# Attention rows scaled before they are turned, with the inverse row sums spread across partitions by two DMA steps

## The chip, the cores and the metric

One core of one Trainium2 chip runs the whole program. The metric is device time in microseconds. The engines are named as in the profile: PE (TensorE, with PEld for its weight loads), DVE (VectorE), ACT (ScalarE), POOL (GpSimd), SP (SyncE, which here only issues DMAs and waits).

## The reference, cut to what matters

Three blocks run one after the other: windowed attention (2 batches, 8 heads, 768 tokens, head dimension 64), a token-mixing and channel MLP, and a gated MLP with a spatial product. The change touches only the end of the attention block and the hand-over to the second block.

```
scores = scale * q @ k^T + bias          # -1e9 outside the window of 96 and the 8 global keys
a = exp(scores - max(scores))
a = a / (sum(a) + 1e-9)
x = (a @ v) as [batch, token, head*dim]
u = x + ((x^T @ U) @ V)^T                # then ch = relu(u @ w_ch1) @ w_ch2; u + ch; the third block
```

## The kernel before

The attention is cut into 24 **quads**: quad g is query tile t = g // 2 (128 queries) with four heads (g % 2 picks which). A tile sees its own block of 128 keys and the block before it (with the global keys copied into it); the first tile of each batch (quads 0, 1, 12, 13) sees one block only. The heads of a quad are held as two pairs m = 0, 1, and within a pair e = 0, 1.

The order is written out by hand: each engine runs a loop over steps s = -2 to 23 (DVE to 24), and in step s handles several quads at different depth.

- PE, step s: `turn(s)` transposes the probabilities of quad s, `turn_o(s-1)` transposes the head outputs of quad s-1, `turn_x(s-2)` transposes the scaled rows of quad s-2 back, `scores(s+2)` makes the scores of quad s+2, then in single steps `gather_z` (s = 13), `fold_z` (14) or a `mix` (15, 17, 19, 21), and `weigh(s)` multiplies with v into `o_bank`.
- DVE, step s: `take_oT(s-1)` copies `o_bank` (dims on partitions, queries along the row) to SBUF, `take_probT(s)` copies half of the turned probabilities, `take_x(s-1)` multiplies the once-turned output in `aux` (queries on partitions) by the inverse sums into `x_all`, `invert(s)` makes the reciprocal of the four sums per query, `score_bias(s+2)` adds the bias and takes the row minimum.
- ACT, step s: `take_probT(s)` (the other half), `add_eps(s+1)` adds 1e-9 to the sums, `take_xT(s-2)` copies the twice-turned output from `aux` into `uT` (dims on partitions), `exps(s+2)` makes the exponentials and their row sums.
- POOL splits the q and k of later quads into high and low parts (`split_qk`) and copies the global keys and values.
- SP loads: `load_qk(t)` issues two DMAs of 256 KB for one tile, `load_v(t)` one. All of them are issued as soon as their buffer is free. After the attention loop it goes on to `load_stage(n)` for the weights from n = 2 on.

So the sums of a query lie on the query's partition, and the output of `weigh` has the dims on partitions; that is why before, the output is turned, scaled and turned again. `x_all` (queries on partitions) is needed for `gather_z`, `uT` (dims on partitions) for all that follows. After step 23 PE runs `hidden(0)`, the first product of the second block; from there to the end 402 us of the span follow.

Of the kernel before, what the change touches and what calls it, by code (L numbers as in the profile page):

```python
# [13 lines left out]
P = 128  # L14
# [11 lines left out]
def build(nc, qk, qT, kT, v, cfg, U, V, w_ch, w_in, w_spT, b_sp, w_out, x_dram, out):  # L26
    B, DM, S = qT.shape
    D = 64
# [22 lines left out]
    with ExitStack() as ctx:  # L51
# [95 lines left out]
        for name, shape, dtype in (("cfg_i", [P, 4], I32), ("cfg_f", [P, 4], F32), ("row_min", [P, 8], F32),  # L147
                                   ("row_sum", [P, 16], F32), ("row_one", [P, 16], F32), ("row_inv", [P, 8], F32),
# [14 lines left out]
        oT = [at(f"oT{r}", [P, 2, P], F32, SLOT * 11 + 2048 + 1024 * r) for r in range(2)]  # L163
# [18 lines left out]
        def sem(name):  # L182
# [15 lines left out]
        sum_eps, inv_ok = sem("sum_eps"), sem("inv_ok")  # L198
        probT_d, probT_a, pv_done, x_half = sem("probT_d"), sem("probT_a"), sem("pv_done"), sem("x_half")
        oT_sb, o_ps = sem("oT_sb"), sem("o_ps")  # L200
        xT_ps, xT_sb, z_acc, z_round, z_split = [sem(n) for n in ("xT_ps", "xT_sb", "z_acc", "z_round", "z_split")]
# [19 lines left out]
            sem("wide_" + n) for n in ("turned", "probT", "out_ps", "o", "store", "back", "heads")]  # L221

# [18 lines left out]
        z_bank, fold_bank = (s_bank[0], aux), (s_bank[2], aux)  # L241

        def mix_bank(j):

            if j < FIRST:

                return s_bank[0]
            return o_bank if j >= 2 * KD and j % 2 else aux

        OT_AMID = (0, 1, 12)
# [112 lines left out]
        def _(sp):  # L365
# [44 lines left out]
            with sp.If(near):  # L410
# [9 lines left out]
                load_v(TILES - 1)  # L420
# [37 lines left out]
        def _(pool):  # L458
# [191 lines left out]
            with pool.If(near):  # L650
# [7 lines left out]
                for g in range(QUADS):  # L658
# [14 lines left out]
                    if g >= 17 and g % 2:  # L673
                        split_u((g - 17) // 2)
# [35 lines left out]
        def _(dve):  # L710
# [62 lines left out]
            def invert(g):  # L773
                sums = row_one[:, g % 4 * 4:g % 4 * 4 + 4]
                dve.wait_ge(sum_eps, g + 1)
                if g >= 2:
                    dve.wait_ge(x_half, g - 1)
                vec.reciprocal(row_inv[:, g % 2 * 4:g % 2 * 4 + 4], sums).then_inc(inv_ok, 1)

            def take_oT(g):  # L780
                dve.wait_ge(pv_done, g + 1)
                if g >= 2:
                    dve.wait_ge(o_ps, g - 1)
                vec.tensor_copy(oT[g % 2][:], o_bank[:, 0:2 * P].rearrange("p (c q) -> p c q", c=2)).then_inc(oT_sb, 1)

            def take_x(g):
                t, hq = divmod(g, 2)
                inv = row_inv[:, g % 2 * 4:g % 2 * 4 + 4]
                dve.wait_ge(inv_ok, g + 1)
                dve.wait_ge(o_ps, g + 1)  # L790
                if g:
                    dve.wait_ge(xT_ps, g)
                if t == XS:
                    dve.wait_ge(z_acc, 1)
                cols = slice(hq * 256, hq * 256 + 256)
                vec.tensor_tensor(x_all[:, t % XS, cols].rearrange("p (h d) -> p h d", d=D),
                                  aux[:, 0:256].rearrange("p (h d) -> p h d", d=D),
                                  inv.unsqueeze(2).to_broadcast([P, 4, D]), ALU.mult).then_inc(x_half, 1)
# [69 lines left out]
            with dve.If(near):  # L868
                for s in range(-2, QUADS + 1):
                    if s >= 1 and s - 1 not in OT_AMID:  # L870
                        take_oT(s - 1)
                    if 0 <= s < QUADS and s != 2:
                        take_probT(s)
                    if s >= 1:
                        take_x(s - 1)
                    if 0 <= s < QUADS:
                        invert(s)
                    if s in OT_AMID:
                        score_bias(s + 2, 0)
                        take_oT(s)  # L880
# [5 lines left out]
                    if s == 14:  # L886
                        split_z(0)
                    if s in (15, 17, 19):
                        sum_u((s - 15) // 2)
                    if s == 22:  # L890
                        sum_u(FIRST - 1)
            with dve.Else():
# [12 lines left out]
                dve.sem_inc(x_half, QUADS)  # L905
# [244 lines left out]
        def _(act):  # L1150
# [19 lines left out]
            def exps(g, half=None):  # L1170
                w = P * blocks(g // 2)
                if g >= 4:
                    act.wait_ge(x_half, g - 3)
# [9 lines left out]
            def add_eps(g):  # L1183
                q = g % 4 * 4
                act.wait_ge(expd, 2 * g + 2)
                sc.activation(row_one[:, q:q + 4], row_sum[:, q:q + 4], ACT.Copy, bias=1e-9).then_inc(sum_eps, 1)

# [7 lines left out]
            def take_xT(g, after=0):  # L1195

                t, hq = divmod(g, 2)
                act.wait_ge(xT_ps, g + 1)
                if after:
                    act.wait_ge(x_half, after)  # L1200
                sc.activation(uT[:, 2 * hq:2 * hq + 2, t * P:(t + 1) * P],
                              aux[:, 2 * P:4 * P].rearrange("p (k t) -> p k t", k=2), ACT.Copy).then_inc(xT_sb, 1)
# [54 lines left out]
            with act.If(near):  # L1257
                for s in range(-2, QUADS):
                    if s >= 3:
                        take_probT(s)  # L1260
                    if s == 13:
                        split_stage(0)
                        copy_z(0)
                    if 0 <= s + 1 < QUADS:
                        add_eps(s + 1)
                    if s == 14:
# [5 lines left out]
                    if s >= 2:  # L1272
# [704 lines left out]
```

## Time and profile before

| | |
|---|---|
| median of 3 runs | 494.83 us (494.77 to 494.99) |
| span of the profiled execution, first to last instruction | 493.2 us |
| PE busy | 489.0 us (99% of the span) |
| DVE, ACT, POOL busy | 310.2, 222.0, 250.2 us |
| granted TensorE clock | 1.000 over the span |

The span leaves out what lies before the first and after the last instruction; the profile gives no time of its own for that, and the median of the runs lies 1.6 us above the span. Busy shares are of the span. Steps of the attention are best read by the start of the same PE instruction in two neighbouring steps.

### The profile page before, as it was taken

To read this page: it belongs to the slowest core of one execution; us is meant where nothing else is said; L and a number is where in the kernel's file an instruction comes from. 1 tells how busy PE (TensorE), PEld (TensorE's weight loads), DVE (VectorE), ACT (ScalarE), POOL (GpSimd) and SP (SyncE) were. 2 spreads that over 40 slices of the span, in tenths; PEclk is the share of its full clock that TensorE was granted. 3 is DMA by queue.
4 is the path that set the end of the run, shared out by engine and by line. 5 is a ranking of instruction groups with operands and counts; after the bars stand their busy time and mean duration, and the time that the engine had idled before them with its cause. 6 is when DMAs were issued, how large, how long until landed. Compare 5 with 4: busy or idle time off the path is not lost.

```text
span 493.2 us, 7961 instructions
## 1 busy us (share of the span) xinstructions
PE 489.0 (99%) x2804; PEld 409.3 (83%) x2804; DVE 310.2 (63%) x727; ACT 222.0 (45%) x520; POOL 250.2 (51%) x221
## 2 busy tenths in 40 slices
PE   9999999999999999999999999999999999999997
PEld 8788677887888888888888888888888888998986
DVE  5888788421279456564655656557868888878600
ACT  7988889532234633242332322415433356333122
POOL 5997576443346666854566546232885201950000
PEclk9999999999999999999999999999999999999999
DMA  8734501132222322012222020220213000001022
GB/s 236 236 127 111 191 2 45 46 128 86 81 87 89 129 85 71 31 72 85 85 86 78 8 85 3 84 64 2 64 65 115 4 0 1 1 1 43 23 85 108
DMA packets 14697, 36.29 MB, mean 74 GB/s; under 512 B 2496, under 2 KB 2752, under 8 KB 14656
## 3 DMA queue, kind: packets, MB, share of 16 engines
q1 hardware_dynamic: 12640, 32.35, 19.8%
q10 hardware_dynamic: 2016, 3.41, 1.8%
q8 instruction: 24, 0.39, 0.3%
q14 instruction: 17, 0.14, 0.1%
HBM read 32.61 MB, written 3.15 MB: 72 GB/s over the span
## 4 chain that ended last, share of the span: by engine, by line
PE 82%; DVE 6%; POOL 4%; ACT 3%; issue 2%; DVEq 2%; DMA 1%; SPq 0%; ACTq 0%
PE bank L1792 15%; PE bank L1724 9%; PE bank L1644 9%; PE bank L1874 8%; PE bank L1821 8%; PE bank L1814 8%; PE bank L1513 7%; PE bank L1551 4%; PE bank L1569 4%; PE bank L1536 4%; PE bank L1503 1%; POOL sp_op L587 1%; PE bank L1583 1%; DVE newton L1020 1%; DVEq L1008 1%
## 5 line engine op out<-in xcount | busy, mean ns | idle before, releaser
L532 POOL TENSOR_TENSOR w_slot<-stage,w_slot 128x1024 fp32r<-128x1024 f32 x30 | 73.0, 2445 | 65.4 <-ACT w_slot L1249 65.4
L940 DVE TENSOR_TENSOR uT<-bank,uT 128x512 f32<-128x512 f32 x68 | 45.8, 689 | 25.2 <-PE bank L1821 23.2
L1179 ACT ACTIVATE prob<-prob,row_min 128x256 f32<-128x256 f32 (+1 forms) x96 | 45.9, 480 | 6.9 <-DVE row_min L756 6.8
L1792 PE MATMUL bank<-u_op,s_slot 128*128 128x512 f32 x192 | 47.6, 389 | 0.0
L1724 PE MATMUL bank<-hid,w_slot 128*128 128x512 f32 x192 | 46.9, 393 | 0.0
L1644 PE MATMUL bank<-u_split,w_slot 128*128 128x512 f32 x192 | 46.5, 391 | 0.0
L1814 PE MATMUL bank<-hid,w_slot 128*128 128x512 f32 x192 | 46.1, 389 | 0.0
L1821 PE MATMUL bank<-hid,w_slot 128*128 128x512 f32 x192 | 46.1, 389 | 0.0
L978 DVE TENSOR_TENSOR part<-part,bank 128x512 f32<-128x512 f32 x40 | 27.4, 686 | 26.9 <-PE bank L1792 26.5
L1724 PEld LDWEIGHTS bank<-hid,w_slot 128*128 128x128 f32 x192 | 35.7, 188 | 8.2 <-issue 0.9
L1814 PEld LDWEIGHTS bank<-hid,w_slot 128*128 128x128 f32 x192 | 36.0, 188 | 7.5
L1821 PEld LDWEIGHTS bank<-hid,w_slot 128*128 128x128 f32 x192 | 36.0, 188 | 7.5
L1792 PEld LDWEIGHTS bank<-u_op,s_slot 128*128 128x128 f32 x192 | 36.0, 188 | 7.5
L1644 PEld LDWEIGHTS bank<-u_split,w_slot 128*128 128x128 f32 x192 | 35.7, 188 | 7.5 <-issue 0.2
L1249 ACT ACTIVATE w_slot<-stage 128x1024 fp32r<-128x1024 f32 x32 | 33.3, 1052 | 12.7 <-DMA stage<-in_w_ch 12.7
L756 DVE CUSTOM_DVE_ANT_0 prob<-bank,bias 128x256 f32<-128x256 f32 (+1 forms) x96 | 32.9, 398 | 6.4 <-PE bank L1536 5.5
L1792 PE MATMUL bank<-u_op,w_slot 128*128 128x512 f32 x144 | 36.5, 389 | 0.0
L950 DVE SCALAR_TENSOR_TENSOR hid<-bank,hid 128x512 fp32r<-128x512 f32 x16 | 11.1, 691 | 39.2 <-ACT hid L1307 39.0
L579 POOL TENSOR_TENSOR s_slot<-s_raw,s_slot 128x1024 fp32r<-128x1024 f32 x8 | 19.2, 2402 | 32.5 <-ACT s_slot L1254 32.5
L1910 PE MATMUL bank<-in_slot,y_split 128*128 128x512 f32 x144 | 32.8, 389 | 0.0
L1513 PE MATMUL bank<-y_split,in_slot 128*128 128x512 f32 x144 | 32.8, 389 | 0.0
L1792 PEld LDWEIGHTS bank<-u_op,w_slot 128*128 128x128 f32 x144 | 27.0, 188 | 5.6
(152 smaller groups left out, 963.5 us busy)
## 6 DMA issues: line engine op xcount, KB each, us to landing
stage<-in_w_ch SPq DMA_DIRECT2D x32, 512.0 KB, 3.3
qk_raw<-in_qk SPq DMA_DIRECT2D x23, 256.0 KB, 4.7
v_all<-in_v SPq DMA_DIRECT2D x12, 256.0 KB, 5.2
out_dram<-o_stage ACTq DMA_DIRECT2D x11, 256.0 KB, 2.0
stage<-in_w_spT SPq DMA_DIRECT2D x6, 384.0 KB, 3.1
stage<-in_w_in SPq DMA_DIRECT2D x4, 512.0 KB, 4.2
stage<-in_w_out SPq DMA_DIRECT2D x2, 512.0 KB, 4.0
V_raw<-in_V SPq DMA_DIRECT2D x4, 96.0 KB, 4.6
```

The costliest lines, as they stand in the source:

```text
L532: nc.gpsimd.tensor_tensor(dst[:, LO, :], stage[n % 2][:, 0:w], dst[:, HI, :].bitcast(F32), ALU.subtract).then_inc(w_lo, 1)
L756: last = vec.tensor_tensor_reduce(prob[r][:, e, 0:w], s_bank[2 * (g % 2) + e][:, m * KC:m * KC + w], bias0[:, h, :] if w == P else bias[:, ...
L940: vec.tensor_tensor(y, y_bank(e)[:], y, ALU.add).then_inc(y_sum, 1)
L1179: last = sc.activation(prob[r][:, e, 0:w], prob[r][:, e, 0:w], ACT.Exp, bias=row_min[:, k:k + 1], scale=-1.0, accum_out=row_sum[:, q:q + 1])
L1249: sc.activation(dst[:, HI, :], stage[n % 2][:, 0:w], ACT.Copy).then_inc(w_hi, 1)
L1513: last = mm(out_ap, lhs(a), rhs(c), start=(n == 0), stop=(n == 3 * len(terms) - 1))
L1644: last = mm(h_bank[f % 2][:], w_slot[f][:, a, k * P:(k + 1) * P], u_split[:, m, k, :], start=(k == 0 and p == 0), stop=(k == KD - 1 and p ...
L1724: last = mm(c_bank[k][:], w_slot[f][:, a, 512 + k * P:512 + (k + 1) * P], hid[f % 2][:, m, :], start=(f == 0 and a == HI and m == HI), sto ...
L1792: last = mm(seven_bank[held][:], lhs, u_op[op][:, m, k, :], start=not more and k == 0 and p == 0, stop=k == 1 and p == 2, skip_group_check ...
L1814: mm(y_bank(e + k)[:], w[r][:, a, 512 + k * P:512 + (k + 1) * P], hid2[r][n][:, m, :], start=(a == HI and m == HI), stop=False, skip_group ...
L1821: last = mm(y_bank(e + k)[:], w[r][:, a, 512 + k * P:512 + (k + 1) * P], hid2[r][n][:, m, :], start=False, stop=(a == LO), skip_group_chec ...
L1874: last = mm(s_banks(q)[held][:, 0:HT], lhs, sp_op[j][:, m, SP_AT[op], :], start=not more and j == 0 and n == 0, stop=j == TC - 1 and n == ...
```

## The change

- `turn_o` and `take_oT` are gone. Quads write alternately into `o_bank` and `aux` (`x_bank(g)`). DVE's `scale_x(g)` multiplies that bank, dims on partitions, by a tile `inv_rows[g % 3]` that holds the inverse sums along the row, the same for all dims of a head, and writes `uT` directly. PE's `turn_x(g)` turns `uT` back into the same bank, and ACT's `take_x(g)` copies it into `x_all`.
- The inverse sums lie on partitions and have to come to lie along the row on all partitions. SP does that through a scratch tensor in device memory: `store_inverse(g)` writes the 128 x 4 values, one element at a time since the target is transposed ("k q -> q k"); `spread_inverse(g)` waits until that has landed and issues two DMAs, each of which reads 2 x 128 values once for each of 64 partitions.
- SP's loads are interleaved with these: in the order store, spread, then `load_qk(g/2 + 4)` after each even quad up to 14, `load_v` at quads 1, 3, and from 11 on, and the first two weight loads at quad 6.
- `add_eps` leaves ACT. DVE's `invert` adds the 1e-9 itself right ahead of the reciprocal, and runs one quad earlier, in step g-1.
- PE's `weigh(g)` now waits for `x_half` of quad g-2 (ACT's `take_x`) instead of `oT_sb` of quad g-1. `gather_z`, `fold_z` and three of the four `mix` sit one step later (14, 15, and 16, 18, 20, 20).

```diff
+            def store_inverse(g):
+                sp.wait_ge(inv_ok, g + 1)
+                sp.dma_start(inv_dram[g, :, :].rearrange("k q -> q k"), row_inv[:, g % 4 * 4:g % 4 * 4 + 4],
+                             allow_slow_non_contiguous=True).then_inc(inv_out[g % 2], 16)
+            def spread_inverse(g):
+                sp.wait_ge(inv_out[g % 2], 16 * (g // 2 + 1))
+                if g >= 3:
+                    sp.wait_ge(xT_sb, g - 2)
+                for e in range(2):
+                    rows = slice(e * D, (e + 1) * D)
+                    sp.dma_start(inv_rows[g % 3][rows, :, :],
+                                 inv_dram[g, 2 * e:2 * e + 2, :].partition_broadcast(D)
+                                 ).then_inc(inv_in[g % 3], 16)
...
-                for t in range(3, TILES):
-                    load_qk(t)
-                    load_v(t - 1)
-                    if t == 6:
+                load_qk(3)
+                load_v(2)
+                load_v(3)
+                for g in range(QUADS):
+                    if g == 11:
+                        load_v(NT)
+                    store_inverse(g)
+                    spread_inverse(g)
+                    if g % 2 == 0 and g // 2 + 4 < TILES:
+                        load_qk(g // 2 + 4)
+                    if g in (1, 3):
+                        load_v((g + 7) // 2)
+                    if g % 2 and g >= 11 and (g + 3) // 2 < TILES:
+                        load_v((g + 3) // 2)
+                    if g == 6:
                         load_stage(0)
                         load_stage(1)
...
             def invert(g):
+                dve.wait_ge(expd, 2 * g + 2)
+                vec.tensor_scalar(row_one[:, q], row_sum[:, q], 1e-9, None, ALU.add).then_inc(sum_eps, 1)
+                if g >= 4:
+                    dve.wait_ge(inv_out[g % 2], 16 * (g // 2 - 1))
                 dve.wait_ge(sum_eps, g + 1)
-                vec.reciprocal(row_inv[:, g % 2 * 4:g % 2 * 4 + 4], sums).then_inc(inv_ok, 1)
+                vec.reciprocal(row_inv[:, q].rearrange("p (e m) -> p m e", e=2),
+                               row_one[:, q].rearrange("p (m e) -> p m e", e=2)).then_inc(inv_ok, 1)
+            def scale_x(g):
+                dve.wait_ge(inv_in[g % 3], 32 * (g // 3 + 1))
                 dve.wait_ge(pv_done, g + 1)
+                vec.tensor_tensor(x_tile(g), x_bank(g)[:, 0:256].rearrange("p (c q) -> p c q", c=2),
+                                  inv_rows[g % 3][:], ALU.mult).then_inc(xT_sb, 1)
...
                 for s in range(-2, QUADS + 1):
-                    if s >= 1 and s - 1 not in OT_AMID:
-                        take_oT(s - 1)
                     if 0 <= s < QUADS and s != 2:
                         take_probT(s)
                     if s >= 1:
-                        take_x(s - 1)
-                    if 0 <= s < QUADS:
-                        invert(s)
+                        scale_x(s - 1)
+                    if 0 <= s + 1 < QUADS:
+                        invert(s + 1)
...
+            def take_x(g):
+                act.wait_ge(x_ps, g + 1)
+                sc.activation(x_all[:, t % XS, hq * 256:hq * 256 + 256], x_bank(g)[:, 0:256],
+                              ACT.Copy).then_inc(x_half, 1)
...
             def weigh(g):
-                if g:
-                    pe.wait_ge(oT_sb, g)
+                if g >= 2:
+                    pe.wait_ge(x_half, g - 1)
...
                     if s >= 0:
                         turn(s)
-                    if s >= 1:
-                        turn_o(s - 1)
                     if s >= 2:
-                        pe.wait_ge(x_half, s - 1)
                         turn_x(s - 2)
```

## Rows read from the trace of the kernel before

**Rows 1.** The page's busy times, then stretches: busy us per engine, granted clock, DMA.
```profile
PE 489.0 (99%) x2804; PEld 409.3 (83%) x2804; DVE 310.2 (63%) x727; ACT 222.0 (45%) x520; POOL 250.2 (51%) x221
...
17.00:45.00 28.00, 27.87 (x324) 23.26 (x326) 23.50 (x98) 24.50 (x96) 26.63 (x37) 1.00 0.38 122
57.00:92.00 35.00, 34.93 (x375) 27.51 (x373) 28.96 (x108) 30.44 (x105) 23.50 (x32) 1.00 0.13 47
```
**Rows 2.** Timeline of PE: start us, us, engine, line, operation.
```profile
36.43 0.44 PE L1583 MATMUL bank<-ident,oT 128*128 128x128 f32 x2
36.71 0.38 PE L1591 MATMUL bank<-ident,x_all 128*128 128x128 f32 x2
37.02 0.97 PE L1536 MATMUL bank<-qk_split 64*128 64x256 f32 x12
37.92 1.09 PE L1569 MATMUL bank<-probT,v_all 128*64 128x128 f32 x16
...
40.48 0.97 PE L1536 MATMUL bank<-qk_split 64*128 64x256 f32 x12
...
92.15 3.02 PE L1644 MATMUL bank<-u_split,w_slot 128*128 128x512 f32 x12
```
**Rows 3.** Timeline of DVE in the same step.
```profile
37.23 0.42 DVE L796 TENSOR_TENSOR x_all<-bank,row_inv 128x256 f32<-128x256 f32 x1 [0.25 <-PE bank L1591]
37.57 0.17 DVE L778 RECIPROCAL row_inv<-row_one 128x4 f32<-128x4 f32 x1
38.03 0.43 DVE L756 CUSTOM_DVE_ANT_0 prob<-bank,bias 128x256 f32<-128x256 f32 x1 [0.30 <-PE bank L1536]
```
**Rows 4.** Timeline of ACT, from this step into the next.
```profile
38.91 0.51 ACT L1179 ACTIVATE prob<-prob,row_min 128x256 f32<-128x256 f32 x1 [0.53 <-DVE row_min L756]
...
40.89 0.58 ACT L1193 ACTIVATE probT<-bank 128x512 f32<-128x512 f32 x1
41.37 0.19 ACT L1186 ACTIVATE row_one<-row_sum 128x4 f32<-128x4 f32 x1
41.46 0.36 ACT L1201 ACTIVATE uT<-bank 128x256 f32<-128x256 f32 x1
```
**Rows 5.** Timeline of ACT at the start.
```profile
9.77 0.18 ACT L1179 ACTIVATION_READ_ACCUMULATOR prob<-prob,row_min 128x1 f32 x1
```
**Rows 6.** DMA issues of the page: KB each, median us from issue to landing.
```profile
qk_raw<-in_qk ACTq DMA_DIRECT2D x1, 256.0 KB, 3.5
out_dram<-o_stage ACTq DMA_DIRECT2D x2, 128.0 KB, 1.7
U_sb<-in_U SPq DMA_DIRECT2D x1, 96.0 KB, 5.2
cfg_i<-in_cfg SPq DMA_DIRECT2D x1, 2.0 KB, 3.0
```
**Rows 7.** The tile v_all: all landings of its loads.
```profile
DMA to landing us min/median/max: 2.6/5.2/6.0
```
**Rows 8.** Timeline of SP: its own time to issue.
```profile
3.54 0.57 SPq L408 DMA_DIRECT2D U_sb<-in_U  x1
...
9.13 0.43 SPq L385 DMA_DIRECT2D v_all<-in_v  x1
...
43.02 0.33 SPq L385 DMA_DIRECT2D v_all<-in_v  x1
43.40 0.91 SPq L377 DMA_DIRECT2D qk_raw<-in_qk  x2
```
**Rows 9.** DMA packets in 7.00 to 8.25 us, then in 451.8 to 452.7 us.
```profile
DMA packets 950, 0.42 MB, mean 338 GB/s; under 512 B 791, under 2 KB 791, under 8 KB 950
...
DMA packets 144, 0.26 MB, mean 291 GB/s; under 512 B 16, under 2 KB 16, under 8 KB 144
```
**Rows 10.** DMA activity from 53.5 to 59.0 us, in 40 slices of 0.14 us, and its issues.
```profile
DMA  0400000289968555236897855678998997662221
...
qk_raw<-in_qk SPq DMA_DIRECT2D x2, 256.0 KB, 3.5
```

More of the change, by code:

```diff
@@ L161, in build @@
         z_part = at("z_part", [P, DM], F32, SLOT * 11)
-        oT = [at(f"oT{r}", [P, 2, P], F32, SLOT * 11 + 2048 + 1024 * r) for r in range(2)]
+        inv_rows = [at(f"inv_rows{r}", [P, 2, P], F32, SLOT * 11 + 2048 + 1024 * r) for r in range(3)]
         pos_w = SLOT * 11 + 2048
@@ L672, in _ @@
                         split_early(1, g // 22)
-                    if g >= 17 and g % 2:
-                        split_u((g - 17) // 2)
+                    for j in range(FIRST):
+                        if g == MIX_AT[j] + 2:
+                            split_u(j)
             with pool.Else():
@@ L885, in _ @@
                         score_bias(s + 2)
-                    if s == 14:
+                    if s == 15:
                         split_z(0)
[L888 to L891, printed above, removed]
+                    for j in range(FIRST):
+                        if s == MIX_AT[j]:
+                            sum_u(j)
             with dve.Else():
@@ L1193, in take_probT, with wide_take_xT @@
                 sc.activation(probT[(2 * g + 1) % 4][:, 0:w], pt_bank[1][:, 0:w], ACT.Copy).then_inc(probT_a, 1)
-            def take_xT(g, after=0):
+            def take_x(g):
                 t, hq = divmod(g, 2)
[L1198 to L1202, printed above, removed]
+                act.wait_ge(x_ps, g + 1)
+                if t == XS and hq == 0:
+                    act.wait_ge(z_acc, 1)
+                sc.activation(x_all[:, t % XS, hq * 256:hq * 256 + 256], x_bank(g)[:, 0:256],
+                              ACT.Copy).then_inc(x_half, 1)
+            def wide_take_xT(g):
+                act.wait_ge(w_xT_ps, g + 1)
+                sc.activation(x_tile(g), x_bank(g)[:, 0:256].rearrange("p (k t) -> p k t", k=2),
+                              ACT.Copy).then_inc(w_xT, 1)
             def copy_z(b):
@@ L1262, in _ @@
                         split_stage(0)
+                    if s == GATHER:
                         copy_z(0)
-                    if 0 <= s + 1 < QUADS:
-                        add_eps(s + 1)
-                    if s == 14:
+                    if s >= 2:
+                        take_x(s - 2)
+                    if s == GATHER + 1:
                         round_z(0)
@@ L1271, in _ @@
                         set_bias(6)
-                    if s >= 2:
-                        take_xT(s - 2, s)
                     if s == 1:
@@ L1282, in _ @@
                         split_stage(1)
-                    if s in (16, 18, 20, 22):
-                        round_u((s - 16) // 2)
+                    for j in range(FIRST):
+                        if s == MIX_AT[j] + 1:
+                            round_u(j)
             with act.Else():
@@ L1294, in _ @@
                 for g in range(2 * NT):
-                    take_xT(g)
+                    wide_take_xT(g)
                 copy_z(0)
@@ L1299, in _ @@
                     round_u(j)
-                for g in range(2 * NT, QUADS - 2):
-                    take_xT(g)
+                for g in range(2 * NT, QUADS):
+                    wide_take_xT(g)
+                act.wait_ge(w_xT, QUADS)
+                act.sem_inc(xT_sb, QUADS)
+                act.sem_inc(x_half, QUADS - 2)
             for f in range(FT):
@@ L1315, in _ @@
                 if f == 0:
-                    take_xT(QUADS - 2, QUADS)
+                    take_x(QUADS - 2)
                 if f == 1:
-                    take_xT(QUADS - 1)
+                    take_x(QUADS - 1)
                 if f == 4:
@@ L1697, in _ @@
                 for g in range(2 * NT):
[L1698 to L1700 removed]
+                    wide_turn_x(g)
                 pe.wait_ge(U_in, 16)
@@ L1711, in _ @@
                 pe.wait_ge(w_back, 16 * TILES)
-                for g in range(2 * NT, QUADS - 1):
-                    pe.wait_ge(xT_sb, g)
-                    turn_x(g)
+                for g in range(2 * NT, QUADS):
+                    wide_turn_x(g)
                 pe.sem_inc(scored, QUADS)
@@ L1717, in _ @@
                 hidden(0)
+                turn_x(QUADS - 2)
             def contract(f):
```

121 lines of the change are left out of this document (51 added, 70 removed).

## The prediction

> **What bounds the kernel now.** First the busy times: PE is busy 99% of the span at a granted clock of 1.00, in the attention too (27.87 of 28.00 us, 34.93 of 35.00) [rows 1]. So the end is set by how much PE has to do, and a saved PE instruction is worth its time as long as nothing else takes its place. Next the timelines of one step, to see how much room the others have. PE needs 40.48 - 37.02 = 3.46 us for a step of two blocks, without a gap: 0.28 `turn_o`, 0.31 `turn_x`, 0.90 `scores`, and 1.97 `weigh` and `turn` together [rows 2]. DVE idles 0.25 ahead of `take_x` and 0.30 ahead of `score_bias`, both for PE [rows 3]; ACT idles 0.53 for DVE's row minimum [rows 4]. Then SP, which has nearly nothing to do before: it issues loads in 0.33 to 0.46 us each and never waits for one to land [rows 8]. `hidden(0)` starts at 92.15 [rows 2]; everything from there on is the same work in both kernels, so the forecast is made on this start.
>
> **What the change takes off.** PE loses two transposes per quad: from the start of `turn_o` to that of `turn_x` 0.28 us [rows 2], times 24 = 6.7 us at most. DVE loses `take_oT` (a copy of 128x256 as large as the 0.42 multiply [rows 3], about 0.34 from start to start, since instructions overlap) and gets a 128x4 add, bounded by the reciprocal's 0.17 from above [rows 3] and nothing from below; I take 0.1. ACT loses 0.09 per quad (41.37 to 41.46) and has a copy of the same size instead of `take_xT` [rows 4]. The multiply now reads its second operand from a full tile rather than a broadcast; same size, same price. `gather_z`, `fold_z`, `mix` only move by a step.
>
> **What it puts on ACT and PE.** `weigh(s)` now waits for `take_x(s-2)`, which ACT runs behind `take_probT(s)`, behind `exps(s+1)`. In the rows, `scores` end and `weigh` starts at 37.92; the exponentials that hang on them start at 38.91, `take_probT` follows at 40.89, the copy would start where `add_eps` stands, at 41.37, and take 0.36 [rows 2, 4]. With 0.11 for a signal (37.92 to DVE's 38.03 [rows 2, 3]) that is 3.92 us after the scores. PE without `turn_o` would be at its next `weigh` after 3.46 - 0.28 = 3.18 us. PE thus waits, and the wait closes a loop over two steps: (3.92 + 3.18) / 2 = 3.55 us per step, against 3.46. So in a plain step of two blocks the 0.28 saved is spent on ACT's copy and 0.09 more; steps with a `gather_z`, `fold_z` or `mix` between scores and `weigh`, and those with one block, keep the saving. Some 14 steps at +0.09 and 10 at -0.28 give -1.5 us; `invert(0)` ahead of `score_bias(1)` makes DVE wait for `exps(0)`, which end at 9.95 [rows 5], about +1 at the start. Without the DMAs the change would be worth about -0.5 us, and -6 at best.
>
> **What it puts on SP.** This is where I expect the time to be decided. SP waits inside its own loop: issue the store, wait until it has landed, issue two reads, then the loads, then the next quad's store. Nothing of the next quad is issued before. One round is
>
> - the store, issue to landing. The nearest row is a 128 KB store, 1.7 us [rows 6]. A 256 KB store moves 144 packets, 0.26 MB, within 0.9 us [rows 9], so about 0.4 of the 1.7 is data and 1.3 is there at any size. This store has 512 elements of 4 bytes, each a write of its own. Nothing before writes so small. `U_sb` is the nearest: of its 128-byte pieces, 791 small packets passed in 1.25 us beside other loads [rows 9], 1.6 ns each, so 512 take 0.8: 2.1 us. Lower bound 1.6 (the elements nearly free). Upper bound from the same load: 768 pieces landed 5.2 us after issue [rows 6], so at most 6.8 ns each, 3.5 for 512: 4.8 us. I take 2.1, since the measured passage is the closer case.
> - a signal, 0.11, and two issues of 0.33 to 0.43 [rows 8], 0.76: together 3.0 us per round.
>
> PE's loop needs scale of quad g only two steps after its inverse, 6.9 us, and one trip is 2.1 + 0.1 + 0.4 + 2.6 (the fastest 256 KB load [rows 7], for a 64 KB read) = 5.2. The latency alone would be hidden, then. But SP's rounds also carry the loads, and these cost twice: their issue, and the queue. Small transfers wait behind large ones of the same queue: `U_sb`, 96 KB, issued at 3.54 behind 256 KB loads, moved only after 7 us and landed after 5.2, where 256 KB alone lands in 2.6 [rows 6, 7, 8, 9]. A load's first packets go about 0.9 after its issue (53.55 to about 54.4, slice 7 [rows 10]) and it is done moving at about 2.3, so a store issued right behind it, which could start 0.9 after its own issue, is held back by 2.3 - 0.43 - 0.9 = 0.95 us, likewise after a pair (issued in 0.91 [rows 8], done at 2.75). The landing of 3.5 in another place [rows 10] would make it 1.85. I take 0.95.
>
> - 22 rounds, quads 0 to 21 (the last that PE needs ahead of `hidden(0)`): 22 x 3.0 = 66
> - eight `load_qk` in them: 8 x (0.91 + 0.95) = 14.9
> - eight `load_v`: 8 x (0.43 + 0.95) = 11.0
> - two weight loads of 512 KB at quad 6: 1 MB at the 338 GB/s of [rows 9] = 3.1
> - the first store stands behind the loads of the start, the last of which was already out at 9.13 before and comes at about 9.6 now [rows 8], and lands with them at about 14.5 instead of 12.5: 2.0
>
> The sum is 97.0 us, 4.4 per quad against PE's 3.46: SP is the new bound, and PE, DVE and ACT wait for `inv_in`. The inverse of quad 0 is ready at 9.95 + 0.45 = 10.4. Then 10.4 + 97.0 = 107.4; the last reads land 2.2 later (second issue at 0.38, 2.6 to land, 0.76 counted): 109.6; `scale_x` 0.53, `turn_x` 0.31, `take_x` 0.47, `weigh` 1.1: 112.0. Before it was 92.15: +19.9 us. On the profiled execution 493.2 + 19.9 = 513.1 us of span; the runs lie 1.6 above it, so 514.7, and I say **515 us**.
>
> **A rule beside it.** The store's fixed part is 1.3 us by [rows 6, 9]. The Trainium skill, page "DMA: Bandwidth & Descriptors", section "Anatomy of one DMA — SWDGE (gpsimd) path", gives some 2.0 us fixed plus bytes over 436 GB/s for a DMA of that path, mostly the receipt of the write; by it the store is 2.0 whatever its pieces, and the sum would be 2 us shorter, 513. The same page, "Rules for kernel authors", says that a strided last dimension lowers to one descriptor per element and should be rearranged; it gives no price per element, and no row here shows such a store.
>
> **The rivals.**
> 1. *Full gain.* If the store takes the lower 1.6 us and small writes slip past the loads, a pair of rounds with a load is 2 x 2.5 + 0.9 = 5.9, under PE's 6.9, and SP is hidden. If ACT also gets `take_x` done in time, because DVE with 0.24 us less to do feeds it earlier, the 6.7 us less 1 at the start come out: 489 us. Against: `U_sb` did not slip past, and DVE's start hangs on `scores`, not on its own work (its 0.30 wait [rows 3]).
> 2. *SP hidden, ACT's copy in the loop.* As 1, but with the 3.55 us step: -0.5, 494.3 us; from 493 to 496 by how many steps keep their saving. For it: the rows of ACT; against: all that speaks for SP's rounds. SP decides from a mean round of 3.5 us on, which is a store of 1.3 us with all the loads' costs, or of 2.6 with none.
> 3. *Costly element writes.* With the store above 3.1 us the sum passes 536 us, and at the upper bound of 4.8 it is 22 x 2.7 = 59 more, 574.
>
> **How the numbers follow.** Forecast 0.54 (its own range 500 to 536: store 1.6 to 3.1 us, loads' queueing from half of what I count to all); costly writes 0.12; ACT's loop 0.15; full gain 0.19. A measurement can tell 0.2%, 1 us. Faster: full gain and about half of case 2, 0.26. Same: 0.07 of case 2. Slower 0.67. The range reaches down to most of the full gain and up to where costly writes begin: 490 to 536.
>
> **What would show it.** Right: SP's own row of waits names the store's landing, about 2 us each, 24 times, and DVE's waits name the spread for `scale_x`, in sum near 20 us; PE's step in 20 to 50 us is 4 to 5 us rather than 3.46, shortest in the late quads without loads; `hidden(0)` starts near 112. `store_inverse` lands in about 2.1 alone and 3 behind a load. The granted clock stays at 1.00; should it fall where PE now has gaps, the time is above mine. Wrong: step 3.2 and no wait for DMA (rival 1), or step 3.55 with PE waiting ahead of `weigh` for ACT's copy into `x_all` (rival 2). The weakest terms are the store's 0.8 us for 512 elements and the 0.95 us behind each load; each 0.1 us on a round is 2.2 us in the end.

## The result, and the profile after

The changed kernel takes 689.4 us (median of 4 runs, 687.5 to 694.0) against 494.8 us: slower by a factor of 1.394, 95% interval 1.390 to 1.399. The forecast was 515 us, range 490 to 536. The direction and the place were right, the size was not: +195 us instead of +20.

The page of the profile after; its line of busy times answers to that of [rows 1]:

```profile
span 692.2 us, 7862 instructions
...
PE 545.1 (79%) x2756; PEld 447.7 (65%) x2756; DVE 305.3 (44%) x727; ACT 219.4 (32%) x496; POOL 250.4 (36%) x221
...
PE 58%; DMA 33%; SPq 6%; ACT 1%; issue 1%; DVE 0%; DVEq 0%; ACTq 0%
DMA inv_scratch<-row_inv 32%; PE bank L1816 11%; PE bank L1541 9%; PE bank L1750 7%; PE bank L1898 6%; PE bank L1838 6%; PE bank L1845 6%; PE bank L1674 6%; PE bank L1934 5%; SPq L412 4%; DMA inv_rows<-inv_scratch 1%; SPq L389 1%; SPq L397 1%; PE bank L1531 1%; ACT prob L1204 1%
```

The last two lines are the chain that ended last, by engine and by line. A third of the span is now a DMA, and nearly all of it is one: the store of the inverse sums into the scratch (`inv_scratch<-row_inv`). The waits and the DMA issues say the same from the other end:

```profile
SPq L412 <- DMA inv_scratch<-row_inv: 217.5, 24, 11.1
...
DVE uT L827 <- DMA inv_rows<-inv_scratch: 215.4, 24, 11.7
...
inv_rows<-inv_scratch SPq DMA_DIRECT2D x48, 64.0 KB, 4.0
inv_scratch<-row_inv SPq DMA_DIRECT2D x24, 2.0 KB, 9.5
```

SP stands 24 times, 217.5 us in all, until a store has landed (L412 is `spread_inverse`; L402 is `store_inverse`, L389 and L397 the loads of q and k and of v), and DVE stands 215.4 us ahead of `scale_x` (L827) for the spread. The store takes 9.5 us from issue to landing. One round of SP, from its timeline:

```profile
43.12 1.09 SPq L412 DMA_DIRECT2D inv_rows<-inv_scratch  x2
44.25 1.06 SPq L389 DMA_DIRECT2D qk_raw<-in_qk  x2
45.35 0.43 SPq L402 DMA_DIRECT2D inv_scratch<-row_inv  x1
55.33 2.12 SPq L412 DMA_DIRECT2D inv_rows<-inv_scratch  x2
```

Store issued at 45.35, the spread of the same quad at 55.33: 10 us in which SP issues nothing else. For the next quad's inverse SP waits once in the whole kernel, 0.8 us, so its rounds run back to back. What the DMA engines do from 48 to 56 us, in 40 slices of 0.2 us:

```profile
DMA  9955210000000000000000000000900000000000
...
DMA packets 614, 0.17 MB, mean 21 GB/s; under 512 B 539, under 2 KB 539, under 8 KB 613
```

The small packets are through by 49.2 us. Then the engines report nothing (one slice of other traffic aside), and the landing comes at 55.3. So the packets themselves are cheap, as I had read from `U_sb`; six microseconds lie behind the last of them. That they are the completion of the writes is a reading: the trace shows only the silence and the landing.

`hidden(0)`, at 92.15 before [rows 2], and what follows it (PE's timeline):

```profile
278.98 4.99 PE L1674 MATMUL bank<-u_split,w_slot 128*128 128x512 f32 x12
283.81 0.38 PE L1610 MATMUL bank<-ident,uT 128*128 128x128 f32 x2
283.94 1.85 PE L1674 MATMUL bank<-u_split,w_slot 128*128 128x512 f32 x7
288.81 1.30 PE L1674 MATMUL bank<-u_split,w_slot 128*128 128x512 f32 x5 [3.02 <-issue]
294.80 0.66 PE L1610 MATMUL bank<-ident,uT 128*128 128x128 f32 x2 [4.69 <-DVE uT L827]
```

It starts 186.8 us later. Another 12.2 us are lost behind it (the spans differ by 199.0), all of them in these rows. The spreads of the last quads are still under way: PE waits 4.69 us for `scale_x`, and 3.02 us for something that the profile does not name. The other 4.5 us are products of the second block that run at a lower clock: the first twelve take 4.99 us instead of 3.02 [rows 2] (granted 0.57 from 278.90 to 284.00 us), the twelve from 295.11 take 5.42 (0.51 from 295.00 to 300.40). From 300.40 on the granted clock is 1.00. Over the attention:

```profile
12.00:290.00 278.00, 139.82 (x868) 105.16 (x868) 63.97 (x276) 69.19 (x239) 61.47 (x84) 0.59 0.22 41
```

The trace agrees in so far as this store of 2 KB takes 9.5 us where one of 128 KB took 1.7 [rows 6]; the size of the writes alone does not explain it, since the experiments below have the same 512 writes done in 2.9 us elsewhere.

### The profile page after: what moved, and what is told of

It is laid out like the page before. It is cut to its first block, busy times and chain, and to the rows that moved or that the text cites. A ratio compares the mean times of both kernels' runs of the same rounds, so it can differ in the third digit from the quotient of the medians.

```text
span 692.2 us, 7862 instructions
## 1 busy us (share of the span) xinstructions
PE 545.1 (79%) x2756; PEld 447.7 (65%) x2756; DVE 305.3 (44%) x727; ACT 219.4 (32%) x496; POOL 250.4 (36%) x221
## 4 chain that ended last, share of the span: by engine, by line
PE 58%; DMA 33%; SPq 6%; ACT 1%; issue 1%; DVE 0%; DVEq 0%; ACTq 0%
DMA inv_scratch<-row_inv 32%; PE bank L1816 11%; PE bank L1541 9%; PE bank L1750 7%; PE bank L1898 6%; PE bank L1838 6%; PE bank L1845 6%; PE bank L1674 6%; PE bank L1934 5%; SPq L412 4%; DMA inv_rows<-inv_scratch 1%; SPq L389 1%; SPq L397 1%; PE bank L1531 1%; ACT prob L1204 1%
## 5 line engine op out<-in xcount | busy, mean ns | idle before, releaser
L827 DVE TENSOR_TENSOR uT<-bank,inv_rows 128x256 f32<-128x256 f32 x24 | 10.2, 424 | 215.4 <-DMA inv_rows<-inv_scratch 215.4
L1610 PE MATMUL bank<-ident,uT 128*128 128x128 f32 x48 | 16.2, 440 | 94.3 <-DVE uT L827 94.3
L1610 PEld LDWEIGHTS bank<-ident,uT 128*128 128x128 f32 x48 | 6.9, 201 | 102.5 <-DVE uT L827 97.2
L1599 PE MATMUL bank<-probT,v_all 128*64 128x128 f32 x352 | 42.0, 411 | 38.2 <-ACT x_all L1221 27.7
L1599 PEld LDWEIGHTS bank<-probT,v_all 128*64 128x64 f32 x352 | 33.2, 214 | 46.8 <-issue 32.5
L1674 PE MATMUL bank<-u_split,w_slot 128*128 128x512 f32 x192 | 48.6, 403 | 3.0 <-issue 3.0
L1750 PE MATMUL bank<-hid,w_slot 128*128 128x512 f32 x192 | 49.4, 408 | 0.0
L542 POOL CAST qk_split<-qk_split 128x128 fp32r<-128x128 f32 x16 | 4.6, 290 | 122.6 <-PE bank L1566 122.6
L1838 PE MATMUL bank<-hid,w_slot 128*128 128x512 f32 x192 | 46.1, 389 | 0.0
L1845 PE MATMUL bank<-hid,w_slot 128*128 128x512 f32 x192 | 46.1, 389 | 0.0
L1674 PEld LDWEIGHTS bank<-u_split,w_slot 128*128 128x128 f32 x192 | 37.3, 197 | 11.4 <-issue 3.6
L1566 PE MATMUL bank<-qk_split 64*128 64x256 f32 (+1 forms) x288 | 36.2, 412 | 7.8 <-DVE uT L840 6.0
L1566 PEld LDWEIGHTS bank<-qk_split 64*128 64x128 f32 x288 | 30.1, 299 | 15.1 <-issue 12.5
```

The costliest lines, as they stand in the source:

```text
L1566: last = mm(s_bank[2 * (g % 2) + e][:, m * KC:m * KC + w], qk_split[rows, a, c, Q, own], qk_split[rows, k, c, K, keys], start=(p == 0), st ...
L1599: last = mm(x_bank(g)[e * D:(e + 1) * D, m * P:(m + 1) * P], v_all[:, i - n + 1 + j, h * D:(h + 1) * D], probT[(2 * g + m) % 4][:, (e * n ...
L1674: last = mm(h_bank[f % 2][:], w_slot[f][:, a, k * P:(k + 1) * P], u_split[:, m, k, :], start=(k == 0 and p == 0), stop=(k == KD - 1 and p ...
L1750: last = mm(c_bank[k][:], w_slot[f][:, a, 512 + k * P:512 + (k + 1) * P], hid[f % 2][:, m, :], start=(f == 0 and a == HI and m == HI), sto ...
L1838: mm(y_bank(e + k)[:], w[r][:, a, 512 + k * P:512 + (k + 1) * P], hid2[r][n][:, m, :], start=(a == HI and m == HI), stop=False, skip_group ...
L1845: last = mm(y_bank(e + k)[:], w[r][:, a, 512 + k * P:512 + (k + 1) * P], hid2[r][n][:, m, :], start=False, stop=(a == LO), skip_group_chec ...
```

## The experiments

### Is it the number of writes, their size, or their place?

**e1_runs16.** The scratch is written in runs of 16 bytes:

```diff
-  inv_dram[g, :, :].rearrange("k q -> q k")
+  inv_dram[g, :, :].rearrange("k q -> (k q)").rearrange("(q k) -> q k", k=4)
```

> The store writes the same 2 KB of a quad as 128 runs of 16 bytes instead of 512 single elements (the scratch then holds them in another order, so the scaling is by misplaced values); all waits and all other transfers are as in the changed kernel. Theory: the landing of the store (9.5 us median in the changed kernel, while its packets move in about 1.2 us) is made of its many small writes, each completed after the other, about (9.5 - 1.3) / 512 = 16 ns each. Then 128 writes land in about 1.3 + 2.0 = 3.3 us, a round of SP is 6.2 us shorter, 22 rounds are 136 us shorter: 553 us. Rival: a write followed by a dependent read through device memory costs its 9.5 us whatever the count of writes: 689 us. Second rival: 16 byte runs go as quickly as full rows, 2.0 us to land: 689 - 22 x 7.5 = 524 us, which would be the sum of the prediction (515) with its store term right.

Measured 536.4 us, ratio 1.083 (1.082 to 1.085): the fixed cost of a trip through device memory is out, and the time lies between the two others, 553 and 524.

**e2_far.** 512 single elements, each in 512 bytes of its own:

```diff
-  inv_dram[g, :, :].rearrange("k q -> q k"), row_inv[:, q4]
+  inv_far[g, :, :, 0:1].rearrange("k q o -> q k o"), row_inv[:, q4].unsqueeze(2)
-  inv_dram[g, 2 * e:2 * e + 2, :].partition_broadcast(D)
+  qT[0, 2 * e:2 * e + 2, 0:P].partition_broadcast(D)
```

> 512 single elements again, but each 512 bytes away from the next in the scratch, so no two fall into one 512 byte line. The two reads that spread the sums take their 2 x 128 values from an input instead (same size and runs), still only after the store has landed, so the scaling is by other values. Theory: the writes queue because they all fall into the same 2 KB, each a partial write of a line that others are also changing; apart they land in 2 to 4 us, total 525 to 565 us. Rival: each small write costs the same wherever it goes: landing 9.5 us, total 689 us.

Measured 537.9 us (one run), within the theory's range of 525 to 565.

**e4_half.** Two of the four columns:

```diff
-  inv_dram[g, :, :].rearrange("k q -> q k"), row_inv[:, g % 4 * 4:g % 4 * 4 + 4]
+  inv_dram[g, 0:2, :].rearrange("k q -> q k"), row_inv[:, g % 4 * 4:g % 4 * 4 + 2]
```

> The store writes only two of the four columns, 256 single elements instead of 512, transposed as before; the reads take these two for both halves, so half of the heads are scaled by sums of others. Theory (cost by count of writes, 16 ns each): landing 1.3 + 4.1 = 5.4 us, round 4.1 us shorter, total 689 - 90 = 599 us. Rival (a fixed cost of the trip through device memory): 9.5 us and 689 us.

Measured 681.4 us (one run). Half the writes save 8 us of 195.

**e12_near4.** Four elements 8 bytes apart, each four in 512 bytes of their own (the edit is shown against e2_far):

```diff
-  inv_far[g, :, :, 0:1].rearrange("k q o -> q k o")
+  inv_far[g, :, 0:8].rearrange("q (k o) -> q k o", o=2)[:, :, 0:1]
```

> As e2_far (512 single elements, the spread reads an input after the store has landed), but the four elements of one query lie 8 bytes apart at the start of a 512 byte piece of the scratch of their own: four writes close together, and 128 such places. In the changed kernel each 512 bytes take 128 single writes, each 64 bytes take 16. If writes wait for each other within some 64 bytes, (9.5 - 2.9) / 15 = 0.44 us for each further one, the store lands at 2.9 + 3 x 0.44 = 4.2 us and the total is 22 x 1.3 = 29 us above e2_far, 567 us. If they wait for each other within 512 bytes, (9.5 - 2.9) / 127 = 0.05 us each, it lands at 3.05 us and the total is 541 us. If four writes from one DMA engine to one place do not queue at all, 2.9 us and 538 us.

Measured 573.8 us (one run), where 567 was forecast for queues of 64 bytes: the landing comes out as forecast, but SP's waits for the store sum to 96.5 us against 61.3 in e2_far, 35 us more where I had 29. The landings of the store in these kernels, from their DMA issues; first e1_runs16:

```profile
inv_scratch<-row_inv SPq DMA_DIRECT2D x24, 2.0 KB, 3.0
```

e2_far:

```profile
inv_scratch<-row_inv SPq DMA_DIRECT2D x24, 2.0 KB, 2.9
```

e4_half:

```profile
inv_scratch<-row_inv SPq DMA_DIRECT2D x24, 1.0 KB, 9.3
```

e12_near4:

```profile
inv_scratch<-row_inv SPq DMA_DIRECT2D x24, 2.0 KB, 4.3
```

Read down: 512 writes land in 2.9 us when they lie apart, 256 in 9.3 when they lie as in the changed kernel. My first theory, 16 ns for each write, falls: e4_half should have been 599 us. What counts is how close together the single writes go. In the changed kernel each 64 bytes take 16 of them, in e4_half also 16, in e1_runs16 four (of 16 bytes), in e12_near4 four, in e2_far one. From 2.9 to 9.5 us for 15 further writes is 0.44 us each; three further ones give 4.2 us, and 4.3 is measured. The other reading, a queue within 512 bytes, would have given 3.05. e1_runs16 fits less directly: four runs per 64 bytes would be 1.3 us above its base, but with 128 packets instead of 512 its base is not that of e2_far. That the place of the writes decides, and not their number, is shown; that close ones wait for each other is the reading that fits. For its size there is only e12_near4: the same arithmetic gives 5.7 us for 32 bytes and 3.5 us for 128, so 64 fits best, if each further write costs the same. One thing changed along with the spacing: in e12_near4 the four writes come from one partition, in the changed kernel the sixteen come from sixteen.

### Does the slow store cost by SP's wait, or also in the queue?

**e11_nowait.** The slow store as it is, but the spread doesn't wait for it:

```diff
-  sp.wait_ge(inv_out[g % 2], 16 * (g // 2 + 1))
-  inv_dram[g, 2 * e:2 * e + 2, :].partition_broadcast(D)
+  qT[0, 2 * e:2 * e + 2, 0:P].partition_broadcast(D)
```

> The changed kernel with its slow store as it is, but nothing waits for it ahead of the spread: the two reads take their 2 x 128 values from an input (same size and runs) and are issued right behind the store. The scaling is by other values. Theory: the 195 us come from SP standing still while the store completes, not from the store's load on the DMA engines, which move its packets in about 2 us and then idle. Then SP's round is some 1.5 us and the time is that of e3_nodma and a little more, 511 to 520 us. Rival: the pending writes also hold up what comes behind them in the queues (the spreads and loads), the spread lands some 9 us after its issue, and the time stays above 600 us.

Measured 605.4 us, ratio 1.222 (1.219 to 1.224). My theory missed by 85 us or more; the rival, a time above 600 us, came true. The waits and issues of this kernel:

```profile
DVE uT L826 <- DMA inv_rows<-in_qT: 113.4, 21, 8.3
...
SPq L402 <- DVE row_inv L819: 120.8, 23, 9.4
...
qk_raw<-in_qk SPq DMA_DIRECT2D x23, 256.0 KB, 11.9
v_all<-in_v SPq DMA_DIRECT2D x12, 256.0 KB, 11.4
```

SP no longer waits for a store, but DVE still waits 113.4 us for spreads issued behind them, and loads that landed in 4.5 and 4.7 us in the changed kernel take 11.9 and 11.4. So what is queued behind these stores is held up too. Taking the dependence away recovers 84 of the 195 us; writing runs of 16 bytes recovers 153, and single elements that lie apart 151.

### Do loads in SP's rounds cost by their data too?

**e9_smallqk.** e1_runs16, the q and k loads of tiles 4 to 11 cut to 16 partitions:

```diff
+  p = slice(0, 16 if t >= 4 else P)
-  sp.dma_start(qk_raw[r][:, c, :, :], qk[t, :, c, :, :])
+  sp.dma_start(qk_raw[r][p, c, :, :], qk[t, p, c, :, :])
```

> As e1_runs16 (store in 16 byte runs), but the q and k loads of tiles 4 to 11 bring only 16 of the 128 partitions, 32 KB instead of 256 KB each; the rest of these tiles is stale q and k. The number of issues is the same. Theory of the prediction: a store right behind a pair of loads is held back about 0.95 us by their data, eight times: 536.4 - 7.6 = 529 us. Rival: a load's cost on SP's round is its issue alone: 536 us as e1_runs16.

Measured 531.0 us, ratio 1.074 (1.072 to 1.075) against 1.083 (1.082 to 1.085): 5.4 us less, 0.7 us per pair of loads where I had 0.95. The store's median landing goes from 3.0 to 2.6 us. The term is there and was somewhat too large; the theory had 529.

### The change without its transfers

**e3_nodma.** No store, no spread, rows multiplied by ones, loads in the order of before:

```diff
-  for g in range(QUADS): store_inverse(g); spread_inverse(g); ...
+  for t in range(3, TILES): load_qk(t); load_v(t - 1); ...
-  dve.wait_ge(inv_in[g % 3], 32 * (g // 3 + 1))
+  vec.memset(inv_rows[r][:], 1.0)      # once, at the start
```

> The change without its transfers: the inverse is still computed but never stored or spread, the rows are multiplied by ones, and SP issues its loads in the order of the kernel before. It leaves out the division by the sums. Theory of the prediction: ACT's copy into x_all closes a loop of 3.55 us over a plain step against 3.46 before, and the total is about the same as before, 494.3 us (493 to 496), with PE waiting ahead of the weigh matmuls for ACT. Rival: ACT keeps up, PE's step is 3.18 us, total 488 to 489 us.

Measured 510.6 us, ratio 1.034 (1.029 to 1.038). I had expected 494. So the new order alone is 16 us slower than the old one, without any of its DMAs. In the changed kernel most of this is covered, since the engines wait there for SP's rounds. Three kernels take the 16 us apart. A good part of them is lost at the start already, as the fourth quad's `weigh` shows in PE's timelines, in the order before, e3_nodma, e6_noinvert, e7_swap:

```profile
20.34 1.45 PE L1569 MATMUL bank<-probT,v_all 128*64 128x128 f32 x16
...
26.99 1.10 PE L1588 MATMUL bank<-probT,v_all 128*64 128x128 f32 x16
...
22.93 1.09 PE L1584 MATMUL bank<-probT,v_all 128*64 128x128 f32 x16
...
21.66 1.09 PE L1584 MATMUL bank<-probT,v_all 128*64 128x128 f32 x16
```

`hidden(0)` starts at 92.15, 107.13, 102.31 and 93.47 in the four. e3_nodma has lost 6.7 of its 15.0 us by the fourth quad, e6_noinvert 2.6 of 10.2.

**e5_noadd.** e3_nodma without the add of 1e-9 on DVE (ACT's wait for the sums becomes one for the reciprocal):

```diff
-  vec.tensor_scalar(row_one[:, q], row_sum[:, q], 1e-9, None, ALU.add)
-  vec.reciprocal(row_inv[...], row_one[...])
+  vec.reciprocal(row_inv[...], row_sum[...])
```

> As e3_nodma (no transfers of the inverse, rows multiplied by ones), and VectorE's 128x4 add of 1e-9 is left out too: the reciprocal reads the sums as they are. What is left out is the division and the 1e-9. Theory: in e3_nodma the add takes 0.16 us when GpSimd is idle or between instructions, but up to 1.4 us when it meets a long GpSimd instruction, since both want the same SBUF port, and the row minimum of the next quad stands behind it, so this is a good part of the 16 us that e3_nodma is above the kernel before. Without it 500 us (498 to 503). Rival: the add only fills time in which VectorE waits for TensorE or ScalarE anyway: 510 us as e3_nodma.

Measured 509.1 us, ratio 1.027 (1.024 to 1.030), an interval that overlaps with that of e3_nodma. A miss: I had expected 500. The add does cost time: the tenth quad's `weigh` starts at 45.79 us here and at 50.67 in e3_nodma, 4.9 us earlier. But `hidden(0)` starts at 107.38, no earlier than there, and most of the gain goes after 90 us, where the granted clock is 0.75 in this execution and 1.00 in that of e3_nodma. The same eight transposes of a `turn`, e3_nodma first:

```profile
95.74 1.09 PE L1570 MATMUL bank<-ident,prob 128*128 128x128 f32 x8
...
92.95 1.97 PE L1568 MATMUL bank<-ident,prob 128*128 128x128 f32 x8
```

So the totals of these kernels differ by their granted clocks too. From 52 to 90 us e5_noadd and e6_noinvert have 0.96, the kernel before, e3_nodma and e7_swap 1.00.

**e6_noinvert.** e3_nodma without `invert`, neither add nor reciprocal:

```diff
-  if 0 <= s + 1 < QUADS: invert(s + 1)
-  act.wait_ge(sum_eps, g - 3)
```

> As e3_nodma, without invert at all: neither add nor reciprocal, and so no wait of VectorE for the exponentials of the quad that invert needs one step earlier than before. What is left out is the whole division. It is the bound for every way to spread the sums. Theory of ACT's loop (3.55 us per plain step against 3.46): 494 to 496 us, against e5_noadd the wait of invert ahead of the row minimum shows as 3 to 6 us. Rival: nothing waits for ACT's copy into x_all, 488 to 489 us.

Measured 505.3 us, ratio 1.022 (1.020 to 1.025): 5.3 us below e3_nodma, but still 10 above before, where I had expected 494 to 496.

**e7_swap.** e6_noinvert, ACT's two copies swapped:

```diff
+  if s >= 2: take_x(s - 2)
   if s >= 3: take_probT(s)
-  if s >= 2: take_x(s - 2)
```

> As e6_noinvert, but ScalarE copies the turned rows into x_all ahead of its half of the turned probabilities, not behind. If ACT's copy into x_all is what holds TensorE ahead of the weigh matmuls, it comes 0.5 us earlier, the loop closes at (3.45 + 3.18) / 2 = 3.3 us per plain step, and the total falls to 489 to 491 us. Rival: the order is of no account, the same as e6_noinvert.

Measured 496.6 us, ratio 1.004 (1.002 to 1.005): 8.7 us below e6_noinvert, and above the 489 to 491 that I had expected. How much of the 8.7 is the order itself and how much the clock, which is 1.00 in its whole attention, was not separated. The starts of `weigh` in PE's timeline, e6_noinvert first:

```profile
26.94 1.09 PE L1584 MATMUL bank<-probT,v_all 128*64 128x128 f32 x16 [0.77 <-ACT x_all L1206]
...
30.11 1.09 PE L1584 MATMUL bank<-probT,v_all 128*64 128x128 f32 x16
...
34.12 1.09 PE L1584 MATMUL bank<-probT,v_all 128*64 128x128 f32 x16 [0.77 <-ACT x_all L1206]
...
98.16 1.09 PE L1584 MATMUL bank<-probT,v_all 128*64 128x128 f32 x16 [2.70 <-ACT x_all L1206]
```

e7_swap:

```profile
28.36 1.09 PE L1584 MATMUL bank<-probT,v_all 128*64 128x128 f32 x16
...
31.89 1.09 PE L1584 MATMUL bank<-probT,v_all 128*64 128x128 f32 x16 [0.28 <-ACT x_all L1206]
...
35.06 1.09 PE L1584 MATMUL bank<-probT,v_all 128*64 128x128 f32 x16
```

In e6_noinvert two steps take 34.12 - 26.94 = 7.18 us, alternately 3.17 (PE alone, forecast 3.18) and 4.01 (PE waits for `x_all`): 3.59 per step against the forecast 3.55, and against 3.46 before [rows 2]. In e7_swap it is 3.17 and 3.53, mean 3.35. That is ACT's loop over two steps as it was forecast, though only with `invert` away: in e3_nodma the six steps from 26.99 to 50.67 take 3.95 us each. What I had left out are the steps where ACT has other work ahead of the copy: at 98.16 PE waits 2.70 us instead of 0.77, and two `round_u`, which took ACT 1.04 us from 96.03 on, are part of that.

**e8_runs16_noadd.** e1_runs16 with the edit of e5_noadd (the first two lines are the store of e1_runs16):

```diff
-  inv_dram[g, :, :].rearrange("k q -> q k")
+  inv_dram[g, :, :].rearrange("k q -> (k q)").rearrange("(q k) -> q k", k=4)
-  vec.tensor_scalar(row_one[:, q], row_sum[:, q], 1e-9, None, ALU.add)
```

> As e1_runs16 (store in 128 runs of 16 bytes, the rest of the transfers as in the changed kernel), without the 128x4 add. Left out: the 1e-9 and the right places of the sums. Theory: SP's rounds bound this kernel, so VectorE's add lies in the shade of its wait for the spread: 535 us, within 2 us of e1_runs16. Rival: the 43 us over the kernel before are mostly the engines' own order, and the total falls by as much as e5_noadd does against e3_nodma.

Measured 538.8 us, ratio 1.089 (1.086 to 1.093). That is 2.3 us more than e1_runs16, not less, and the two intervals do not meet. The rival, a gain as that of e5_noadd, is out: where SP's rounds bound the kernel, the add is covered. Why leaving it out costs 2.3 us stays open.

### The add alone, in the kernel before

**e10_before_add.** The kernel before, 1e-9 added by DVE:

```diff
-  dve.wait_ge(sum_eps, g + 1)
+  dve.wait_ge(expd, 2 * g + 2)
+  vec.tensor_scalar(sums, row_sum[:, g % 4 * 4:g % 4 * 4 + 4], 1e-9, None, ALU.add).then_inc(sum_eps, 1)
+  dve.wait_ge(sum_eps, g + 1)
-  if 0 <= s + 1 < QUADS: add_eps(s + 1)      # ACT
```

> One part of the change alone: the kernel before, with the 1e-9 added by VectorE right ahead of its reciprocal, instead of by ScalarE, all else as before. Nothing is left out. Theory: in the kernel before VectorE has 0.55 us to spare per step, the add takes 0.16 us when the port is free and up to 1.4 us beside a long GpSimd instruction, so some steps are prolonged: 496 to 499 us. Rival: the spare time hides it: 494.8 us. Second rival: the 0.09 us less on ScalarE shortens nothing, since TensorE sets the step, and the add costs nothing either: the same.

Measured 498.9 us, ratio 1.0075 (1.0061 to 1.0089), at the upper end of the 496 to 499 forecast: this part alone costs 4.1 us. The grouped rows of the two small DVE instructions in it:

```profile
L778 DVE TENSOR_SCALAR row_one<-row_sum 128x4 f32<-128x4 f32 x24 | 9.1, 379 | 0.0
...
L780 DVE RECIPROCAL row_inv<-row_one 128x4 f32<-128x4 f32 x24 | 4.3, 178 | 0.8
```

and one add of e3_nodma in DVE's timeline, beside POOL's:

```profile
37.73 1.42 DVE L808 TENSOR_SCALAR row_one<-row_sum 128x4 f32<-128x4 f32 x1 [0.56 <-ACT prob L1193]
39.18 0.18 DVE L810 RECIPROCAL row_inv<-row_one 128x4 f32<-128x4 f32 x1
```

```profile
37.30 1.81 POOL L554 TENSOR_TENSOR V_stack<-V_raw,V_stack 32x768 fp32r<-32x768 f32 x1
```

An add of four elements per partition takes 1.42 us and ends 0.04 us behind POOL's instruction; the fastest in e3_nodma takes 0.158. This is no single case: the eleven adds of e3_nodma that took 0.53 us or more all end 0.02 to 0.04 us behind a POOL instruction that ran when they began. The reciprocal, as small, never varies (177 to 179 ns in e3_nodma). The Trainium skill, "SBUF — State Buffer", "Who interferes with whom", has it: `tensor_scalar` can run in a mode that takes the port pair that VectorE shares with GpSimd, and then it waits until a GpSimd instruction that got the pair first is over. The trace agrees, with 0.379 us on average in e10_before_add, where the fastest took 0.156.

## Why the prediction was right and wrong

- **SP's rounds are the new bound.** Right. The chain runs through them, DVE waits for the spread in all 24 quads, SP's own row of waits names the store 24 times. The forecast had about 2 us for each and some 20 us for DVE's waits in sum; they are 9.1 and 215.4.
- **The store, issue to landing: 2.1 us.** This is the term that failed: 9.5 us. The 22 rounds give 22 x 7.4 = 163 us, which with the 19.9 forecast makes 183 of the 186.8 us that `hidden(0)` moved. The upper bound of 4.8 was no bound: it came from `U_sb`, small pieces read from device memory and written to 128 partitions. Those never meet in one place in device memory. The packets here are through early too (by 49.2 us of a landing at 55.3); the landing of the store, with 16 writes to each 64 bytes, comes six us behind them. The rule beside the sum, 2.0 us whatever the pieces, fails by the same 7.5 us. Rival 3, costly element writes, was the right one and had 0.12; its price was capped by the same bound.
- **The rest of the sum.** With the store of e1_runs16, 3.0 us, the forecast's sum is 515 + 22 x 0.9 = 535 us, measured 536.4. Part of this agreement is luck: 3.0 is the median over all 24 stores, so it counts what loads add a second time. The eight stores right behind a bare spread land there in 2.1 to 3.4 us, 2.5 on average; with that the sum is 524, 12 us short. Two terms that were too small make it up. The two reads of a spread are issued in 1.09 us instead of 0.76, 7.3 us over 22 rounds. And from the last of these rounds to `hidden(0)`, at 133.26, 9.8 us pass instead of 4.6. One term was too large: behind a v load the store lands in 2.8 us on average, 0.3 more than alone instead of 0.95. SP's rounds run without a break in e1_runs16 (one wait of 1.0 us for an inverse), but DVE waits for the spread in 17 quads only, 33.0 us in all.
- **The loads' data behind a store.** 0.7 us instead of 0.95 per pair (e9_smallqk). In the changed kernel the eight stores behind a q and k pair (one of them with weight loads between, one with a v load) land in 10.5 us on average (8.55 to 11.56), the seven right behind a bare spread in 9.2 (7.80 to 10.45): 1.3 us. From its chain, one of either kind (L389 is the pair's issue, L412 the spread's):

```profile
68.40 0.43 SPq L389
68.87 10.95 DMA inv_scratch<-row_inv
79.84 0.45 SPq L412
80.33 0.60 SPq L412
80.98 9.27 DMA inv_scratch<-row_inv
```

- **Everything from `hidden(0)` on is the same.** Off by 12.2 us: the last two quads' spreads come behind it (7.7 us of waits of PE), and its first products run at a lower granted clock (4.5 us).
- **DVE's add at 0.1 us with the reciprocal as upper bound.** Wrong in kind: 0.16 free, 0.38 on average in the order of before, up to 1.4. Where SP's rounds bound the kernel it is covered (e8_runs16_noadd); alone it costs 4.1 us. None of the rows of before has such an instruction, so they gave no price for it.
- **ACT's loop, 3.55 us per plain step.** Right with `invert` away, 3.59; with it a plain step of e3_nodma takes 3.95. **Without DMAs -0.5 us.** Wrong: +15.8. The start was put at +1 us and costs 6.7, of which 4.1 go with `invert` (e6_noinvert). In sum `invert` is worth 5.3 us; its add, its reciprocal and its place one quad earlier were not told apart. Swapping ACT's two copies gives back 8.7 us (e7_swap). Steps with other work on ACT ahead of the copy and dips of the granted clock, which none of these kernels but e7_swap is free of, are both in that; their shares stay open.
- **The full-gain rival, 489 us.** Even with no inverse at all and ACT's copies in the better order the time is 496.6 us, above the kernel before. So a faster way to spread the sums would not, by itself, have made this order faster than before. Whether a further reordering would bring the transposes' 6.7 us out was not tried.
- **The granted clock stays at 1.00.** Wrong, 0.59 in the attention. The forecast named this case as one in which the time is above its own. Up to `hidden(0)` SP's rounds set the time, and they wait for an inverse only once, 0.8 us; behind it the lower clock costs 4.5 us.

## What to carry to other kernels

A DMA that writes single elements transposed into device memory is to be priced by how close together they fall, and an estimate from small reads or from small writes that lie apart is no bound. A store that the issuing queue waits for, with the loads in the same queue, makes that queue a serial engine: sum its rounds before anything else, and expect slow writes to delay what is queued behind them too. And a tiny VectorE instruction is not free beside a busy GpSimd: the add cost 4.1 us when it was moved there from ScalarE, which had 0.09 us per quad for it. When an experiment takes work away and the time does not fall, look at the granted clock of the stretch before calling the work free.

## What the runs showed of the hardware

- 512 writes of 4 bytes into device memory land in 2.9 us when 512 bytes apart, 4.3 us with four of them within 32 bytes, 9.5 us with sixteen per 64 bytes (9.3 us for half as many, laid out alike).
- The DMA engines report no work for about 6 us of such a store, and yet loads queued behind such stores land in 11.9 us instead of 4.5 (e11_nowait).
- A VectorE `tensor_scalar` on 128x4 SBUF values takes 0.16 us, or as long as the GpSimd instruction beside it has still to run (1.4 us at most); a reciprocal of the same size is untouched, 0.18 us each time.
- The granted clock of TensorE fell to 0.59 on average in the attention of the changed kernel, where PE was busy half of the time. The same eight transposes took 1.97 us in e5_noadd where they took 1.09 in e3_nodma.
